# Convolution and two feed-forward layers on one core: order of VectorE's and ScalarE's work at a tile's change-over, and the place of the later softmax sums

## The reference

```
w = softmax over the 7 taps of weight_gen            # 8 heads, per token
x = sum over k of w[k] * x_padded[token + k]         # causal convolution, 24 channels per head
h = max(x @ w_in, 0);   x = (h * h) @ w_out          # 192 -> 2048 -> 192
h = x @ w_in2;          x = (h * cos(h)) @ w_out2    # 192 -> 2048 -> 192
```

## Time and profile before

| | |
|---|---|
| median of 3 runs | 1189.62 us (1189.56 to 1189.83) |
| profiled execution, own time | 1189.38 us |
| its span, first to last instruction | 1187.6 us |
| TensorE matmuls busy | 1170.7 us (99%) |
| VectorE busy | 962.7 us (81%) |
| ScalarE busy | 808.1 us (68%) |
| GpSimd busy | 366.8 us (31%) |
| mean granted TensorE clock | 0.999 |
| DMA | 37.32 MB, mean 31 GB/s |

### The profile page before, as it was taken

How to read it: one execution, slowest core, us unless ns; L and a number is a source line. 1 busy time by engine, 2 the same in 40 slices (tenths; PEclk the granted TensorE clock), 3 DMA queues, 4 the chain that set the end, 5 groups by cost and what they waited for, 6 DMA issues and landing times.

```text
span 1187.6 us, 25485 instructions
## 1 busy us (share of the span) xinstructions
PE 1170.7 (99%) x9800; PEld 1101.7 (93%) x9800; DVE 962.7 (81%) x1506; ACT 808.1 (68%) x1467; POOL 366.8 (31%) x265
## 2 busy tenths in 40 slices
PE   6999999999999999999999999999999999999998
PEld 5989998899999999999999999999999999999976
DVE  7978888878778787787878878787787878878787
ACT  4877666767666676676667666676666767666675
POOL 3995524070330705115070330705215070000000
PEclk9999999999999999999999999999999999999999
DMA  6512111101111101111001111101111000100000
GB/s 187 143 45 48 35 28 34 17 16 35 25 34 28 35 9 20 34 28 34 15 15 38 24 35 28 34 9 20 34 28 34 14 16 4 25 2 14 1 15 15
DMA packets 113173, 37.32 MB, mean 31 GB/s; under 512 B 101662, under 2 KB 110878, under 8 KB 113052
## 3 DMA queue, kind: packets, MB, share of 16 engines
q1 hardware_dynamic: 111100, 34.87, 14.0%
q10 hardware_dynamic: 1952, 0.80, 0.3%
HBM read 23.84 MB, written 6.29 MB: 25 GB/s over the span
## 4 chain that ended last, share of the span: by engine, by line
PE 91%; DVE 5%; ACT 2%; issue 1%; SPq 0%; DMA 0%; ACTq 0%; DVEq 0%
PE y L598 47%; PE h L598 43%; DVE h L1429 1%; DVE h L1450 1%; DVE g_lo L1462 1%; DVE turns L1435 1%; ACT turns L1138 1%; ACT g_hi L1151 1%; DVE x L1406 0%; DMA xc<-in_x_dram 0%; DVE stat L1285 0%; DVE stat L1276 0%; DVE turns L1315 0%; DVE g_lo L1473 0%; DVE tap L1352 0%
## 5 line engine op out<-in xcount | busy, mean ns | idle before, releaser
L598 PE MATMUL y<-g_hi,wo 64*128 64x512 f32 x3048 | 697.2, 395 | 0.6 <-DVE y_part L1485 0.4
L598 PE MATMUL y<-g_lo,wo 64*128 64x512 f32 x2032 | 524.4, 392 | 0.0
L598 PEld LDWEIGHTS y<-g_hi,wo 64*128 64x128 f32 x3048 | 421.9, 184 | 28.4 <-PE y L598 4.9
L519 POOL TENSOR_TENSOR tap<-xc,gen 128x768 f32<-128x768 f32 x98 | 151.4, 1551 | 582.0 <-DVE xd_lo L1479 566.4
L598 PEld LDWEIGHTS y<-g_lo,wo 64*128 64x128 f32 x2032 | 307.8, 184 | 5.8
L1138 ACT ACTIVATE turns<-turns 128x512 f32<-128x512 f32 x238 | 150.4, 632 | 196.8 <-DVE turns L1435 196.0
L598 PE MATMUL h<-xa_hi,wa_hi 64*128 64x512 f32 x1018 | 273.5, 399 | 0.6 <-DVE g_lo L1473 0.4
L598 PE MATMUL h<-xa_lo,wa_hi 64*128 64x512 f32 x1018 | 269.8, 393 | 0.4 <-DVE g_lo L1320 0.3
L598 PE MATMUL h<-xa_hi,wa_lo 64*128 64x512 f32 x1018 | 268.4, 391 | 0.0
L1450 DVE TENSOR_TENSOR h<-h,turns 128x512 f32<-128x512 f32 x238 | 165.8, 696 | 122.5 <-ACT turns L1138 121.6
L1429 DVE SCALAR_TENSOR_TENSOR h<-h,relu 128x512 f32<-128x512 f32 x249 | 173.2, 696 | 61.4 <-ACT relu L1114 59.2
(11 more groups left out here) (122 smaller groups left out, 1083.8 us busy)
## 6 DMA issues: line engine op xcount, KB each, us to landing
xc<-in_x_dram SPq DMA_DIRECT2D x60, 240.0 KB
out_dram<-arena SPq DMA_DIRECT2D x62, 64.0 KB, 1.9
xt_a<-x_blocks SPq DMA_DIRECT2D x224, 16.0 KB, 1.8
arena<-in_moe_w_out_dram SPq DMA_DIRECT2D x16, 192.0 KB, 3.2
arena<-in_moe_w_in_dram SPq DMA_DIRECT2D x16, 128.0 KB, 2.5
out_dram<-arena SPq DMA_DIRECT2D x62, 32.0 KB, 1.7
xt_d<-x_blocks SPq DMA_DIRECT2D x112, 16.0 KB, 1.8
arena<-in_moe_w_in_dram SPq DMA_DIRECT2D x16, 64.0 KB, 3.0
```

The source lines that it names most:

```text
L519: pool.tensor_tensor(tap[:, k % 2, :].rearrange("p (r g) -> p r g", g=GROUP), rows[k], wk, ALU.mult).then_inc(pool_step, 1)
L598: return pe.matmul(o, w[rows, :], x[rows, :], start=start, stop=stop)
```

## The change

- In the slot i = 1, `x2_high` and `x2_low` are each cut in two. The halves for channels 0 to 127 (`x2_high_a`, `x2_low_a`) now stand ahead of ScalarE's sine and of VectorE's product with the cosine. The halves for channels 128 to 191 (`x2_high_d`, `x2_low_d`) go to the end of the slot. At t = 16 (i = 0) the second halves stay where they were, and at t = 1 nothing moves.
- In the slot i = 4, `turn_y2_a` (L1300) stands ahead of VectorE's product with the cosine.
- A second table, `SOFTMAX_IN`, places softmax pieces between VectorE's fraction and its product. The pieces of parts 3 to 8 go into it: at n = 29, 30, and then at 38, 39, 41, 42, 43, 44, 45, 46, 47 and 54, so that i = 8 of tile 2 stays free.

```diff
--- before.py
+++ after.py
@@ -269,8 +269,10 @@
         LOADS = [0, 2, 5, len(PARTS) - 1]
         SOFTMAX_AFTER = {0: [(1, 2), (1, 3), (1, 4)]}
         SOFTMAX_AFTER.update({n: [(n - 1, 0)] for n in range(3, 10)})
-        SOFTMAX_AFTER.update({12: [(2, 2)], 13: [(2, 3)], 29: [(3, 2)], 30: [(3, 3)]})
-        SOFTMAX_AFTER.update({2 * SLOTS + 6 + k: [(4 + k // 2, 2 + k % 2)] for k in range(10)})
+        SOFTMAX_AFTER.update({12: [(2, 2)], 13: [(2, 3)]})
+        SOFTMAX_IN = {29: [(3, 2)], 30: [(3, 3)]}
+        SOFTMAX_IN.update({2 * SLOTS + (6, 7, 9, 10, 11, 12, 13, 14, 15, SLOTS + 6)[k]: [(4 + k // 2, 2 + k % 2)]
+                           for k in range(10)})
         EXPS_AFTER = {n: n - 8 for n in range(10, 17)}
         COPIES_AFTER = [STEPS - 11, STEPS - 7, STEPS - 3, STEPS]
         SIN_AFTER = 16
@@ -1128,6 +1130,7 @@
                     x1_highs(t, par)
                 if i == y1_at(t) and t > 1:
                     x2_part(t, par)
+                    x2_high_a(t, par)
                 if i == Y2_AT and tile_live(t - 2):
                     act.wait_ge(y2_d_done, SLOTS * (t - 1))
                     if counted(t - 2):
@@ -1137,8 +1140,8 @@
                     act.wait_ge(fraction_ready, m + 1)
                     act.activation(wave[:, c, :], wave[:, c, :], ACT.Sin,
                                    scale=2.0 * math.pi).then_inc(cos_ready, 1)
-                if i == y1_at(t) and t > 1:
-                    x2_high(t, par)
+                if i == y1_at(t) and t == TILES:
+                    x2_high_d(t, par)
                 if live(n) and m != 0:
                     high(n)
                 if i == split_at(t) and t == 0:
@@ -1151,7 +1154,9 @@
                     act.activation(g2_hi[:, c, :], h2[c], ACT.Copy, scale=2.0 * math.pi).then_inc(g2_hi_ready, 1)
                 if i == Y1_AT and t == 1:
                     x2_part(t, par)
-                    x2_high(t, par)
+                    x2_high_a(t, par)
+                if i == y1_at(t) and 0 < t < TILES:
+                    x2_high_d(t, par)
 
             def high(n):
 
@@ -1174,13 +1179,16 @@
                 act.activation(y1_part, first_sums(t - 1)[0:DD, 1, :], ACT.Copy,
                                scale=INV_2PI).then_inc(y1_part_ready, 1)
 
-            def x2_high(t, par):
+            def x2_high_a(t, par):
 
                 act.wait_ge(down1_done, SLOTS * t)
                 if counted(t - 2):
                     act.wait_ge(up2_done, SLOTS * (t - 2))
                 act.activation(xa_hi[1][:, 1 - par, :], first_sums(t - 1)[:, 0, :], ACT.Copy,
                                scale=INV_2PI).then_inc(x2_hi_ready, 1)
+
+            def x2_high_d(t, par):
+
                 act.wait_ge(y1_summed, t)
                 act.activation(xd_hi[DD:P, 1 - par, :], y1_part, ACT.Copy).then_inc(x2_hi_ready, 1)
                 if t == TILES:
@@ -1443,16 +1451,19 @@
                     turn_y2_d(t - 2)
                 if i == Y2_AT and tile_live(t - 2):
                     add_y2_d(t - 2, y2)
+                    turn_y2_a(t - 2, y2)
                 if i == y1_at(t) and t > 1:
                     sum_y1(t)
+                    x2_low_a(t, par)
+
+                for part, op in SOFTMAX_IN.get(n, ()):
+                    softmax(part, op)
                 if live(m):
                     dve.wait_ge(cos_ready, m + 1)
                     dve.tensor_tensor(h2[c], h2[c], wave[:, c, :],
                                       ALU.mult).then_inc(g2_made, 1)
-                if i == Y2_AT and tile_live(t - 2):
-                    turn_y2_a(t - 2, y2)
-                if i == y1_at(t) and t > 1:
-                    x2_low(t, par)
+                if i == y1_at(t) and t == TILES:
+                    x2_low_d(t, par)
                 if live(n) and m != 0:
                     low(n)
                 if i == split_at(t) and t == 0:
@@ -1485,11 +1498,14 @@
                 dve.scalar_tensor_tensor(y1_part, first_sums(t - 1)[DD:P, 1, :], INV_2PI, y1_part, ALU.mult,
                                          ALU.add).then_inc(y1_summed, 1)
 
-            def x2_low(t, par):
+            def x2_low_a(t, par):
 
                 dve.wait_ge(x2_hi_ready, 2 * t - 1)
                 dve.scalar_tensor_tensor(xa_lo[1][:, 1 - par, :], first_sums(t - 1)[:, 0, :], INV_2PI,
                                          xa_hi[1][:, 1 - par, :], ALU.mult, ALU.subtract).then_inc(y1_read, 1)
+
+            def x2_low_d(t, par):
+
                 dve.wait_ge(x2_hi_ready, 2 * t)
                 dve.tensor_tensor(xd_lo[DD:P, 1 - par, :], y1_part, xd_hi[DD:P, 1 - par, :],
                                   ALU.subtract).then_inc(x2_split, 1)
```

## The result

| | before | changed |
|---|---|---|
| median | 1189.63 us (1189.43 to 1189.83, 6 runs) | 1181.97 us (1181.63 to 1182.28, 6 runs) |
| ratio, 95% interval | | 0.9935 (0.9923 to 0.9948) |
| profiled execution's own time; span | 1189.38; 1187.6 us | 1182.28; 1180.5 us |

The change takes 7.66 us off the median, where 6.3 were forecast: faster by 0.65%, inside the range and near its fast end. In the profiled executions it is 7.10 us. TensorE's slots i = 2, 5, 6 and again 2, which answer to the earlier trace rows, read as follows in the timeline of the changed kernel. (By the count of the adds in the earlier trace rows, the stretch from 349 us on, and the one that the prediction calls tile 4, is tile 5. Nothing rests on the name.)

The account below looks back on a forecast made before the run. TensorE's matmuls cover 1170.7 of 1187.6 us; late VectorE loses 0.43 us a tile at change-overs. 14 tiles at 0.35 (4.9) plus softmax 1.4 give 6.3 us off 1189.38; median 1183.3 us, range 1181.5 to 1187.0.

Parts of the forecast that it names:

- Part 1: Reordering slot i = 1 removes TensorE's waits for xa_lo in slot 2 and g2_lo at slot 3: 0.35 us per tile.
- The distance between VectorE's rows: Neighbouring VectorE rows in the replay of i = 1 were allowed 0.60 to 0.73 us, the two distances seen.
- the return at slot 4: Loss coming back when slot 4 wants g2_lo earlier: taken as 0.02 us, 0 if every end takes its early value.
- that wait goes: Slot 2's load no longer waits 0.20 us for xa_lo (`y1_read`), with 0.58 us to spare.
- What is late next: After slot 3, g2_lo at slot 4 and the add for slot 5 lack reserve; 0.02 and 0.06 us come back.
- Part 2: At i = 4, L1300 starts 0.73 us earlier, so slot 5's loss of 0.08 us per tile goes.
- Part 3: Softmax pieces moved into VectorE's hole before the product win 1.4 us, bounds -0.7 and 2.1.
- GpSimd's hold: Moved softmax additions at n = 30, 42 and 44 may wait for GpSimd: 0 to 2.4 us lost, 0.35 taken.
- The waits only move on: Rival, chance 0.18: VectorE has no reserve behind slot 2, TensorE wins only 0.12 us a tile; 1186.5 us.
- GpSimd did hold three additions: Rival, chance 0.10: three softmax additions wait a whole 1.85 us in the slot, each costing 0.8 us; 1185.3 us, or 1187.
- xd_lo was in time: Rival, chance 0.05: slot 3's fourth pair waits for the later xd_lo, losing 0.5 us a tile; 1195.2 us.
- No effect: Rival, chance 0.07: matmul distance or the ring of y_part copy, add and `d_first` paces the kernel; 1189.4 us.

Follow-up runs that it names:

- xd_left: Changed kernel, but xd_hi and xd_lo (channels 128 to 191) stay behind sine and product at i = 1; 1183.05 us.
- i4_only: Kernel before with only `turn_y2_a` (L1300) moved ahead of the product at i = 4; slot i = 1 and softmax table as before; 1187.06 us.
- xa_left: Changed kernel, but xa_hi and xa_lo (channels 0 to 127) stay behind sine and product, xd_hi and xd_lo at the slot's end; 1181.42 us.
- i1_only: Kernel before with only slot i = 1 reordered; L1300 and softmax pieces as before; 1188.19 us.
- sum_in_hole: Changed kernel plus 110 VectorE sums of 0.61 us between fraction and product, ten slots in each of tiles 4 to 14; 1181.95 us.
- no_hold: Changed kernel with softmax additions and reciprocals of parts 5 to 8 placed where GpSimd has no convolution; 1182.04 us.
- add_in_hole: Changed kernel plus 50 VectorE additions of 0.19 us between fraction and product, slots 9 to 13 of tiles 4 to 13, beside GpSimd's convolution; 1182.90 us.

## Why the prediction was right, and where it was off

- **Part 1, the two waits of slots 2 and 3.** Both went. The replay held: y_part to g2_lo 2.69 us (2.70 to 2.83 forecast), to the next square 4.13 (4.04 to 4.24). xd_lo ends at 353.99, and slot 3's fourth pair, whose load starts at 354.41, was never kept waiting.
- **The distance between VectorE's rows.** The product follows xa_lo by 0.60 us (350.62 to 351.22), the early value, as the rule in the Trainium skill's "VectorE: DVE Perf Modes", section "Two Vector instructions with no wait between them", had it. The next step, that by this rule every end takes its early value, misread it. xd_lo begins at partition 64, in another group of 32 than its neighbours, so the rule has it held, and the square behind it too. The trace agrees: they come 0.72 us behind the row before them (352.58, 353.30, 354.02). With that the square comes 0.09 us later than by early values alone (4.13 against 4.04), and the return at slot 4 was not 0 but 0.05 us.
- The step "that wait goes" for y1_read credited xa_lo's move with a gain. It has one only where xd stays (xd_left against i4_only, 0.12 us a tile). Beside xd's move it has none: xa_left keeps that wait and its tile is shorter. Here the prediction put down the right sum to one cause too many.
- **What is late next.** The worry was sound, as i1_only shows: without part 2 the wait only moves to slot 5. With it, slots 2 to 5 take 17.81 us (17.73 to 17.85 forecast).
- **Part 2** was undersized within the sum. 0.08 us per tile was slot 5's own loss; i4_only wins 0.19 per tile, since the lanes' distance goes too. That 0.1 us was booked among the 0.35 of slots 2 to 4. In the sum it makes no difference, since both stand in the 0.43. What the sum had too large is the return: 0.08 us taken, 0.04 measured over the tile (70.97 against 70.93). The gain per tile was 0.39 us, not 0.35: 14 x 0.39 = 5.5 us instead of 4.9.
- **Part 3.** Of the 1.68 us, 1.6 went: tile 2 is 1.98 us shorter, 1.59 without its 0.39. The stretch before it, with the pieces of n = 29 and 30, is 0.15 shorter (68.27 to 68.12 us between adds of y_part). This second figure is not firm: xd_left and sum_in_hole, which have the same pieces there, take 67.86 and 67.87. Together they are 1.74 us instead of 1.4. The mis-sized term is the 0.35 us for GpSimd's hold. The waits came as named, at n = 30, 42 and 44, up to 1.55 us long, longer than the one of 1.34 us seen before. But I charged the whole wait against the room before `g2_ready`, and the hole, which was idle anyway, takes its part first. no_hold puts the price at 0.08 us in tile 2. The upper bound of 2.1 us has no working: the terms give 1.78.
- **Sum.** 5.5 + 1.74 = 7.2 us, the profiled executions' 7.10; the medians differ by 7.66. The last 0.56 us are no mechanism of the forecast: the profiled execution was the slowest of the changed kernel's six runs, and 0.25 us below the median in the kernel before.
- **The rivals.** "The waits only move on" is true of i1_only and not of the whole. GpSimd did hold three additions, two of them for over 1 us, and that cost next to nothing. xd_lo was in time, with 0.4 us to spare. "No effect" fell with the measured time; the plain slot stayed at 4.43 us.

## What to carry to other kernels

An engine that is idle inside its chain, waiting for another engine's answer, takes small work there at no cost (110 sums of 0.61 us, 67 us in all, and no loss), while the same work at the end of a step adds up until it meets the first deadline without room. When several waits come one behind the other, take them away together and measure each part alone and in pairs: here 1.3 and 2.4 us alone were 5.4 together. Then try the halves of a part, alone and beside the rest: xa's move won 0.12 us a tile alone and nothing beside xd's.

## What was not expected of the hardware

- **Two lanes keep their distance.** After a wait that stops one of the two 64-row streams of matmuls, they stayed 0.15 us apart for twelve slots (pairs of 0.54 us instead of 0.39 to 0.44), and that cost 0.1 us at the next change-over. In i4_only, without that wait, they stay 0.05 to 0.06 apart. Such a wait is not the only source: in the changed kernel the distance grows from 0.06 us in slot 5 to 0.15 in the next slot 1, and why is open. A wait that stops both brings them together (0.39), and a kernel with such a wait of 0.20 us a tile was faster by 0.5 to 0.7 us than one without it. How much of that is the distance, and how much the changed kernel's wait at slot 4, was not tried.
- A VectorE addition of 0.19 us lasts up to 1.55 us beside GpSimd. In add_in_hole 45 of the 50 lasted 0.25 us or more, and each of these ended 0.05 to 0.06 us behind an instruction of GpSimd. The sums of 0.61 us never grew: 50 of the 110 in sum_in_hole ran beside GpSimd's convolution.
